# Loads of a chunked mLSTM with two mixture layers: SyncE issues the lower queries and values before the keys, and on ScalarE's event

## The reference

```
m_new = max(f_t + m, i_t);  fs = exp(f_t + m - m_new);  is = exp(i_t - m_new)
C = fs * C + is * v_t k_t^T;   n = fs * n + is * k_t
y_t = sigmoid(o_t) * (C q_t) / max(|n . q_t|, 1)
```

## Time and profile before

| | |
|---|---|
| median of three runs | 278.94 us (278.02 to 280.15) |
| the profiled execution | 279.06 us |
| its span, from the first to the last instruction | 277.3 us |
| PE busy | 247.5 us, 89% of the span |
| DVE busy | 181.4 us, 65% |
| ACT busy | 87.5 us, 32% |
| POOL busy | 65.4 us, 24% |
| mean granted TensorE clock | 0.993 |
| moved by DMA | 54.73 MB, 197 GB/s over the span |

### The profile page before, as it was taken

How to read it: one execution, slowest core, us unless ns; L and a number is a source line. 1 busy time by engine, 2 the same in 40 slices (tenths; PEclk the granted TensorE clock), 3 DMA queues, 4 the chain that set the end, 5 groups by cost and what they waited for, 6 DMA issues and landing times.

```text
span 277.3 us, 7971 instructions
## 1 busy us (share of the span) xinstructions
PE 247.5 (89%) x3264; PEld 205.3 (74%) x3264; DVE 181.4 (65%) x460; ACT 87.5 (32%) x143; POOL 65.4 (24%) x100
## 2 busy tenths in 40 slices
PE   0459989789897999999899998999699999999995
PEld 0448888678786998988579445666456679999995
DVE  6972778848685778887459324646958877444550
ACT  3568601212222132233151033534400023434341
POOL 9412152414241434266301313310000000000000
PEclk9999999999999999999999999999899999999999
DMA  7968999999999877501999999940000001222222
GB/s 237 354 154 292 249 236 245 264 267 285 249 298 258 214 208 203 163 3 20 401 415 420 426 420 448 396 191 0 2 0 0 0 2 47 95 93 74 95 83 87
DMA packets 22436, 54.73 MB, mean 197 GB/s; under 512 B 4000, under 2 KB 14400, under 8 KB 21248
## 3 DMA queue, kind: packets, MB, share of 16 engines
q1 hardware_dynamic: 18320, 50.24, 54.1%
q10 hardware_dynamic: 4080, 3.98, 5.8%
HBM read 49.99 MB, written 4.23 MB: 196 GB/s over the span
## 4 chain that ended last, share of the span: by engine, by line
PE 71%; DVE 17%; DMA 4%; issue 3%; SPq 2%; ACT 1%; DVEq 0%
PE ps L982 61%; DVE attn L742 4%; PE ps L1198 4%; DMA attn<-kk 4%; PE ps L1073 3%; PE ps L1079 2%; DVE attn L754 1%; SPq L435 1%; DVE attn L755 1%; DVE xreg L768 1%; PE ps L1204 1%; DMA xTreg<-ig 1%; DVE attn L725 1%; ACT freg L607 1%; DVE xTreg L698 1%
## 5 line engine op out<-in xcount | busy, mean ns | idle before, releaser
L982 PE MATMUL ps<-attn 128*64 128x41 f32 (+3 forms) x2016 | 89.5, 248 | 8.4 <-issue 3.0
L982 PEld LDWEIGHTS ps<-attn 128*64 128x64 f32 (+1 forms) x2016 | 83.1, 136 | 16.3 <-issue 7.5
L501 POOL TENSOR_TENSOR attn<-attn 128x160 f32<-128x160 f32 x48 | 21.1, 460 | 74.1 <-issue 55.4
L742 DVE SCALAR_TENSOR_TENSOR attn<-attn,small,ps 128x41 f32<-128x41 f32 x176 | 30.9, 249 | 4.4 <-PE ps L982 4.4
L982 PE MATMUL ps<-woreg,tlow 128*128 128x320 f32 x96 | 28.2, 457 | 2.5 <-DVE tlow L932 2.5
L982 PE MATMUL ps<-Whr,Phr 128*128 128x320 f32 x96 | 30.0, 313 | 0.0
L982 PE MATMUL ps<-Whr,Plr 128*128 128x320 f32 x96 | 29.7, 309 | 0.0
L982 PE MATMUL ps<-Wlr,Phr 128*128 128x320 f32 x96 | 29.6, 309 | 0.0
L585 ACT COPY xTreg<-ps 128x512 f32<-128x512 f32 x22 | 12.7, 588 | 53.4 <-PE ps L1073 53.4
L982 PEld LDWEIGHTS ps<-woreg,tlow 128*128 128x128 f32 x96 | 18.5, 200 | 11.9 <-DVE tlow L932 4.6
L725 DVE TENSOR_TENSOR attn<-ps,attn 128x512 f32<-128x512 f32 x24 | 16.5, 688 | 10.5 <-issue 5.7
(11 more groups left out here) (161 smaller groups left out, 343.1 us busy)
## 6 DMA issues: line engine op xcount, KB each, us to landing
attn<-kk SPq DMA_DIRECT2D x24, 416.0 KB, 7.7
front<-w SPq DMA_DIRECT2D x10, 512.0 KB, 9.9
tail<-w SPq DMA_DIRECT2D x10, 512.0 KB, 8.4
xTreg<-w SPq DMA_DIRECT2D x4, 1280.0 KB, 14.0
xreg<-og SPq DMA_DIRECT2D x4, 960.0 KB, 7.4
xreg<-w SPq DMA_DIRECT2D x3, 1280.0 KB, 12.1
front<-wab SPq DMA_DIRECT2D x1, 3840.0 KB, 15.8
out<-tlow SPq DMA_DIRECT2D x24, 160.0 KB, 1.8
```

The lines of the kernel that those rows point to most:

```text
L501: last = g.tensor_tensor(ksb[n % 2][:, c, 0:HU * D].rearrange("r (h e) -> r h e", h=HU), knb[n % 3][:, c], last_col[:, c].unsqueeze(2).to_ ...
L742: last = v.scalar_tensor_tensor(out=C[:, cc + 1, p], in0=C[:, cc, p], scalar=dcy[:, 2 * u + p, cc:cc + 1], in1=pUv[:, p, c, 0:VW], op0=ALU ...
L982: return t_.matmul(o_, l_, r_, start=start, stop=stop)
```

## The change

`load_block` issues the same three DMAs with the same buffers, in another order. The lower queries come first. From block 4 on they wait for `e_sb >= n - 1` (the exponential of block n - 2 is finished; ACT issues the upper halves right behind starting it), for `x_ps` as before and for `s_ps >= n - 3`. The lower values follow, with the waits that they had. The keys are last, with the waits that they had.

```diff
             def load_block(n):
                 u, blk = n // NBLK, n % NBLK
                 t0, tn = blk * CB * L, CB * L
-                if n >= 3:
-                    sp.wait_ge(s_ps, n - 2)
-                    sp.wait_ge(ks_sb, n - 2)
-                sp.dma_start(kkb[n % 3], kk[u, blk]).then_inc(ld_k[n % 3], 16)
                 if n >= NQ:
+                    sp.wait_ge(e_sb, n - 1)
                     sp.wait_ge(x_ps, n - NQ + 1)
+                    sp.wait_ge(s_ps, n - NQ + 1)
                 sp.dma_start(qb[n % NQ][0:D, :, 0, :], qT[u, 0, :, :, t0:t0 + tn]).then_inc(ld_q[n % NQ], 16)
                 if n >= NQ:
                     sp.wait_ge(u_ps, n - NQ + 1)
                     sp.wait_ge(y_ps, n - NQ + 1)
                 sp.dma_start(vb[n % NQ][0:64, 0, 0:2 * HU * VW], v1[u, 0:64, blk, :]).then_inc(ld_v[n % NQ], 16)
+                if n >= 3:
+                    sp.wait_ge(s_ps, n - 2)
+                    sp.wait_ge(ks_sb, n - 2)
+                sp.dma_start(kkb[n % 3], kk[u, blk]).then_inc(ld_k[n % 3], 16)
```

## The result

The changed kernel takes 280.75 us (median of 10 runs, 279.0 to 282.45) against 278.77 us before on the same chip (276.7 to 280.15). The ratio is 1.0088, with a 95% interval of 1.0053 to 1.0122. By the medians that is 2.0 us slower, by the ratio 2.5 us. Some executions of a kernel are slower than its others as a whole; the ratios in this document leave them out, the medians do not. The change is less than the 1% that the prediction called distinguishable, but clear of zero with this many runs. The profiled execution took 281.13 us with a span of 279.3 us, 2.1 us more than that of before. The forecast was 280.4 us.

A forecast was written before the change was run, and what follows sets the result against it. The prediction took the volume of loads to bound the kernel from 38 to 94 us. Its terms, 0.7 + 0.8 + 0.3 - 0.3 = +1.5 us on 278.94, gave 280.4 us, range 277.4 to 284.3.

The forecast's parts named there:

- The bound: From 38 to 94 us the volume of loads sets the pace: 1252 KB a block at 263 GB/s, 4.87 us.
- The keys' new issue time and window: Keys issued 2.1 us behind the start of exponential n - 2, leaving 6.2 us to land, 7.6 in the full stretch.
- a count of 7.0: Full stretch: w1 piece 2.0, queries and values 1.3, keys 1.6, DMA start and end 2.1 us make the landing.
- Block 1: Keys of block 1 issued later and landing later, delaying its scores: +0.7 us, bounds 0 and 1.6.
- The lag is not made up in the stretch: The lag from the start stays until the w1 pieces end, as landings run at the pace of the DMA engines.
- Queries and values in front of the keys: Scores wait for keys that now also follow the lower values (82 KB): +0.3 us once, not per block.
- The lost lead: Keys of blocks 4 to 7 come 3 to 5 us later, DMA partly idle: +0.8 us, bounds 0 and 2.0.
- SP held by w1: Issues of w1 pieces on SP, up to 3.54 us, shrink with a shorter queue: -0.3 us, bounds -1.1 and +1.
- The rule of the Trainium skill: Queries on 40 partitions use only ten DMA engines, 84.3 KB per block against a mean of 78.3: 280.7 us.
- The slower one: Full stretch: keys land in 8.7 us, missing 7.6; period 5.4, ten blocks cost 5.3 us, about 284.3 us; chance 0.20.
- The prediction's own sign for it: DMA share in the full stretch below 0.95 with PE idle at each score would mean slower.
- the faster one: PE gaps before and within scores, 4.8 us, mostly go: 275.3 us; chance 0.10; sign: above 263 GB/s in full stretch.

The follow-up runs named there:

- the spread of w1: The kernel before, with the ten w1 pieces issued behind every second block (5 to 23) instead of blocks 6 to 15: 274.37 us, ratio 0.9884.
- either half: Kernel before plus one of two edits: lower queries wait for the exponential, keys first (0.9947); or from block 4 queries, values, keys without that wait (0.9967).
- the late gates: The changed kernel, with the last output gates (960 KB) moved behind the loads of block 3: 286.77 us, ratio 1.0253.
- the event from block 6: The changed kernel, with the lower queries waiting for the exponential from block 6 on only: 281.33 us, ratio 1.0118.
- the keys of block 1 first: The changed kernel, with the keys of block 1 issued in front of its queries and values as before: 279.02 us, ratio 1.0040.
- from block 4 on alone: The kernel before, with the changed order and the wait for the exponential from block 4 on only: 279.41 us, ratio 1.0013.
- the transposes: The changed kernel, with ten transposes of the identity on TensorE just ahead of the scores of block 1: 280.53 us, ratio 1.0091.
- the event alone: The kernel before, keys still first, with only the lower queries and values behind them waiting for the exponential of block n - 2: 276.91 us, ratio 0.9947.
- the new start alone: The kernel before, with the order queries, values, keys for blocks 0 to 3 only: 277.88 us, ratio 0.9999.
- the pair above: The kernel before with the new order for blocks 0 to 3 alone (0.9999) and with order and event from block 4 on alone (1.0013); together 1.0088.

## Why the prediction was right, and which terms were off

*The bound.* That the stretch from block 6 to 16 is set by its loads was borne out by the spread of w1 (4.22 us a block in place of 4.87). That its pace is a fixed 263 GB/s was not: it ran at 4.62 us with 270 GB/s in the whole change and at 272 to 274 GB/s with either half of it.

*The keys' new issue time and window.* The issue time was right, 2.1 to 2.4 us behind the start of exponential n - 2; the light stretch stayed hidden, 3.3 to 5.3 us from issue to landing. In the full stretch landing fell from 11.7 to 7.1 us in the median of the first execution traced, against a window of 7.6 and a count of 7.0. That was a favourable one. Five other traced executions run the same steady part beside the full stretch, and their medians and periods were 7.6 us and 4.59 (the late gates), 8.3 and 4.79 (the event from block 6), 8.3 and 4.80 (the keys of block 1 first), 8.5 and 4.87 (from block 4 on alone), 8.5 and 4.92 (the transposes). So in four of them the landings missed the window, and PE waited for keys eight to eleven times, 6.0 to 8.4 us in all. The miss was cheap, because the prediction priced it wrongly: it took (landing + 2.1) / 2 for the period, which gives 5.3 at 8.5 us. But scores that are late by w also put off the next exponential by w, so the period is 4.13 + w. Counted from exponential n - 2, scores n begin after two periods and w, and that is landing + 2.1. Together, 3 x period = landing + 2.1 + 4.13: the loop spans three periods, and a microsecond too much costs a third of one, not half. At 7.6, 8.3 and 8.5 us that estimate gives 4.61, 4.84 and 4.91; the first execution does not fit it as well, 4.44 at 7.1 us against its 4.62, but its landings reached up to 9.1. At the rival's 8.7 it gives 4.98, about 1.1 us over ten blocks and not 5.3. No run changed the landing time by itself, and the volume gives 4.87 as well, so this shows a relation, not which of the two leads.

*Block 1.* The right mechanism, and the term that was mis-sized most: 0.7 us, with a bound of 1.6, against a wait of 2.55 us. The landing took 4.97 us and not the 3.1 to 4.0 of the rows that I took it from, the issue was another 0.5 us later, most of it a longer wait for `scratch_b`, and the clock then added 1.5 us. In the runs with the same start the wait was 0.64 to 2.97 us, so its size varies by execution.

*The lag is not made up in the stretch.* Wrong in the profiled execution: a start that was 3.9 us late was 1.4 us late at block 16. In the others the lag between blocks 6 and 16 went from 1.35 to 0.2, from 1.1 to 0.4, from 4.6 to 3.8, from 8.1 to 5.4, and with the transposes from 1.8 up to 2.3; so part of it is mostly made up, by an amount that varies by execution. This error and the one before are opposite, and that is why the sum of +1.5 us stood so close to the +2.1 of the profiled execution and the 2.5 of the ratio. It was right by luck in its size, not by its parts. The bounds of the terms, too, add up to -0.8 and +4.9, not to the +0.3 and +3.3 that were given.

*Queries and values in front of the keys.* The 0.3 us was isolated by no run.

*The lost lead.* Right in kind: the share from 23 to 38 us fell from 0.97 to 0.69. I had it from the later issues of blocks 4 to 7 alone; much of it lies beside one gap of 5.5 us on SP, because the keys of block 4 stand behind queries that wait for a late `carried(0)` and then for the exponential. Alone, the new order from block 4 on costs 0.1%.

*SP held by w1.* Its longest issue fell from 3.54 to 1.36 us. The term of -0.3 is too small, if the gain of the event alone, 0.5%, is of this kind; these runs don't separate it from the gaps without a name. The rule of the Trainium skill by which the queries use ten engines ("DMA: Bandwidth & Descriptors", section "Why a DMA increments its semaphore by 16 and not by 1") gave 280.7 us. No run settles it, and that the measured 280.75 lies so near is chance, as the other terms of that sum missed. By that rule the mean share could hardly pass 78.3 / 84.3 = 0.93 in a stretch set by its loads (an estimate from the page's rule and the prediction's bytes); it was 0.98 before and 0.99 in the run with the new start alone, which speaks against the rule here, though the view is not exact, as shares of 1.02 and 1.04 stand in it too.

*The rivals.* The slower one, landings over the window, occurred: in part in the profiled execution (up to 9.1 us, seven waits of PE beside block 1's), fully in the four named above. It cost far less than its 5.3 us. The prediction's own sign for it, a share below 0.95 with PE idle at each score, came close to true in the change from block 4 on alone: 0.94 from 38 to 94 us, 0.95 from 45 on. The prediction's sign for the faster one, more than 263 GB/s, came true in the profiled execution (270) while the kernel got slower, so it was not a good sign. That the gaps which this rival named can be had back is what the halves of the change point to, 0.9 to 1.5 us by their ratios.

*Still open:* what PE's gaps without a name are, and why either half removes them. The trade of these gaps for waits on keys is what separates the halves from the two together, in one trace each. The depth of the queue would order the cases too (11.5 us of landing before, 9.9 and 9.7 with one half, 8.5 with both from block 4 on), but the whole change, with 7.1 us, had 270 GB/s again, and no run changed the depth by itself.

## What to carry to other kernels

If a stretch is bound by the volume of its loads, look first at what in it could be loaded elsewhere: spreading ten pieces that are needed much later gave 1.2%, more than any order of the issues, and with either half of this change 1.8 to 2.0%. Such a stretch can absorb a good part of a late start of the compute engines. Idle time of the DMA engines ahead of it seems to be what it does not absorb; that is the reading of the pair above, not a measurement. So keep early the load with the fewest waits, and be slow to put it behind one whose buffer comes free later. When you price a load that misses its window, count the periods that the loop through it spans: here three, where the prediction had two. And one traced execution is not the kernel: the period of the same stretch of code was 4.59 to 4.92 us in six of them. Changes of a steady order should be checked at the first blocks by themselves, where there is no lead to live on.

## What the runs showed of the hardware

A DMA stream in use at full share does not move at one rate: from 38 to 94 us, in nine of the ten traces with the w1 pieces in that stretch, shares of 0.93 to 0.99 went with 261 to 274 GB/s, and the highest rate was not at the highest share (0.97 with 274, 0.99 with 267). The same steady code ran at 262, 263, 265 and 270 GB/s in four executions.

Gaps of 1.86, 2.13, 2.55 and 2.97 us on TensorE, all in front of the scores of block 1, were each followed by a granted clock of 0.50 to 0.58 from 28 to 30 us. A gap of 0.64 us was not, and with ten transposes in the gap, of which 1.31 us were left, the clock stayed at 1.00.

The same key load, issued at the same place, landed in 4.2, 4.4, 4.97 and 5.1 us in four executions. With 4.2 the clock did not fall, with 4.97 and 5.1 it did, and the one of 4.4 had the transposes.
